# Retention scores with the key halves of odd chunks exchanged in PSUM, and three steps placed elsewhere

## What is computed

```python
def _attn_ref(q, k, v):                      # q, k, v: (2, 8, 768, 64)
    gamma = 1.0 - 2.0 ** (-5.0 - arange(H))
    for t in range(S):
        state = gamma * state + k[t] (outer) v[t]
        y[t] = q[t] @ state / sqrt(D)

def _moe_ref(x, g_ln, w_ch1, w_ch2):         # x: (2, 768, 512), y with its heads side by side
    xn = (x - mean(x)) / sqrt(var(x) + 1e-6) * g_ln
    return x + relu(xn @ w_ch1) @ w_ch2
```

## Time and profile before

| what | value |
|---|---|
| median of 3 executions | 446.19 us (446.08 to 446.53) |
| profiled execution, its own time | 447.54 us |
| span of the profiled execution | 445.8 us |
| TensorE busy | 439.6 us, 99% of the span |
| VectorE busy | 316.7 us, 71% |
| ScalarE busy | 227.5 us, 51% |
| GpSimd busy | 291.4 us, 65% |
| granted TensorE clock | 1.00 of full speed |

### The profile page before, as it was taken

The page is one execution under the profiler, slowest core; times in us unless marked ns, Lnnn a source line. Parts: engine busy times, 40 slices in busy tenths (PEclk is TensorE's granted clock), DMA queues, the critical chain, the costliest instruction groups (busy, mean ns, idle before and its releaser), DMA issues.

```text
span 445.8 us, 8757 instructions
## 1 busy us (share of the span) xinstructions
PE 439.6 (99%) x3150; PEld 400.0 (90%) x3150; DVE 316.7 (71%) x670; ACT 227.5 (51%) x531; POOL 291.4 (65%) x390
## 2 busy tenths in 40 slices
PE   7999999999999999999999999999999999999997
PEld 7899988989898899898989898988999999999886
DVE  2655889767876857776786677648557888887963
ACT  3458965532451465444245234215436777777853
POOL 2856845989788599997876696632803355566650
PEclk9999999999999999999999999999999999999999
DMA  8999304221211311331132260020163533333214
GB/s 206 253 264 258 119 0 143 56 84 50 96 51 49 91 33 63 94 96 48 49 94 62 81 164 4 0 49 1 25 152 78 141 94 97 93 97 89 89 49 165
DMA packets 68474, 41.52 MB, mean 93 GB/s; under 512 B 35792, under 2 KB 62672, under 8 KB 68432
## 3 DMA queue, kind: packets, MB, share of 16 engines
q1 hardware_dynamic: 66288, 40.37, 33.3%
q10 hardware_dynamic: 2144, 0.60, 0.6%
HBM read 28.37 MB, written 3.15 MB: 71 GB/s over the span
## 4 chain that ended last, share of the span: by engine, by line
PE 95%; DVE 1%; DMA 1%; ACT 1%; issue 1%; ACTq 0%; DVEq 0%
PE ps L988 30%; PE ps L969 25%; PE ps L1104 8%; PE ps L1123 4%; PE ps L1157 4%; PE ps L1138 4%; PE ps L1074 4%; PE ps L1193 3%; PE ps L823 3%; PE ps L812 3%; PE ps L835 3%; PE ps L928 2%; PE ps L881 1%; PE ps L848 1%; DMA decay_sb<-decay 1%; PE ps L1086 1%
## 5 line engine op out<-in xcount | busy, mean ns | idle before, releaser
L1388 ACT ACTIVATE h_t_hi<-ps 128x384 fp32r<-128x384 f32 x64 | 31.3, 490 | 126.2 <-DVE ps L1742 68.2
L988 PE MATMUL ps<-w_hi,h_t_lo 128*128 128x512 f32 x192 | 76.1, 397 | 0.0
L988 PE MATMUL ps<-w_lo,h_t_hi 128*128 128x512 f32 x192 | 75.8, 395 | 0.0
L988 PE MATMUL ps<-w_hi,h_t_hi 128*128 128x512 f32 x192 | 74.7, 389 | 0.0
L681 POOL TENSOR_TENSOR w_lo<-raw_w,w_hi 128x512 fp32r<-128x512 f32 x32 | 43.1, 1369 | 40.0 <-ACT w_hi L1335 30.4
L772 POOL TENSOR_SCALAR a<-a,inv_den,weight 128x768 f32<-128x768 f32 (+5 forms) x48 | 34.0, 718 | 52.5 <-DVE inv_den L1984 28.0
L1723 DVE SCALAR_TENSOR_TENSOR h_t_lo<-ps,h_t_hi 128x384 fp32r<-128x384 f32 x64 | 35.6, 556 | 32.6 <-ACT h_t_hi L1388 32.6
L666 POOL TENSOR_TENSOR w_lo<-w_sum,w_hi 128x256 fp32r<-128x256 f32 x60 | 45.1, 762 | 2.4
L988 PEld LDWEIGHTS ps<-w_hi,h_t_lo 128*128 128x128 f32 x192 | 36.0, 187 | 7.7
L1476 ACT ACTIVATE a<-a,neg_max 128x768 f32<-128x768 f32 (+5 forms) x48 | 32.2, 674 | 16.9 <-DVE neg_max L1965 16.9
L969 PE MATMUL ps<-xq_T_lo,w_hi 128*128 128x384 f32 x120 | 40.6, 338 | 0.0
(11 more groups left out here) (206 smaller groups left out, 1193.5 us busy)
## 6 DMA issues: line engine op xcount, KB each, us to landing
raw_w<-in_moe_w_ch SPq DMA_DIRECT2D x64, 256.0 KB, 2.9
k_twice_hi<-pj_hi SPq DMA_DIRECT2D x32, 96.0 KB, 2.2
k_twice_lo<-pj_lo SPq DMA_DIRECT2D x32, 96.0 KB, 2.2
out_y<-out_sb SPq DMA_DIRECT2D x11, 256.0 KB, 2.0
raw_k<-in_k SPq DMA_DIRECT2D x7, 384.0 KB, 5.8
raw_q<-in_q SPq DMA_DIRECT2D x7, 384.0 KB, 5.9
raw_v<-in_v SPq DMA_DIRECT2D x7, 384.0 KB, 5.2
q_both<-pj_hi SPq DMA_DIRECT2D x16, 96.0 KB, 2.1
```

The lines of the kernel that those rows point to most:

```text
L988: mm = pe.matmul(acc_bank(tau), h_tile(a_, m, which)[:, u * P:(u + 1) * P], w2[b_][:, m % 2, part, :], start=(m % NG == 0 and which in ("1 ...
L1388: act.activation(h_tile("hi", m, part), part_bank(m, part), ACT.Relu).then_inc(s_hhi, 1)
```

## The change

1. In `scores_of` the result of key half 0 of an odd chunk goes to PSUM partitions 64 to 127 and that of half 1 to 0 to 63; even chunks stay as they were. Which chunk of a group is odd depends on the group: the middle one in group 0, the outer two in group 1.
2. `apply_causal` becomes three instructions for each group in place of one: one for the even chunks, and for the odd chunks one for each half, which reads the PSUM half on the other side and writes the half of `prob` where it belongs. The block of the odd chunks that is always zero is no longer written there.
3. GpSimd prepares a second form of the triangle in `causal`, and clears the zero block of `prob` with four memsets, before it starts to scale. VectorE waits for this (`s_const` at 10 in place of 4).
4. `scale_last("q")` stands ahead of all four first `weight_lo` in GpSimd's list; it stood between the second and the third.
5. The four `centre` of batch 0 stood ahead of `states(6)`. Now two stand behind `states(6)` and two behind `states(7)`.

```diff
-            pool.memset(causal[:, :], 1.0).then_inc(s_const, 1)
+            pool.memset(causal[:, :, :], 1.0).then_inc(s_const, 1)
             pool.wait_ge(s_const, 3)
...
+            pool.affine_select(out=causal[:, 1, 0:D], in_=causal[:, 1, 0:D], compare_op=ALU.is_ge, fill=0.0, base=D,
+                               pattern=[[1, D]], channel_multiplier=-1).then_inc(s_const, 1)
+            pool.affine_select(out=causal[0:D, 1, D:P], in_=causal[0:D, 1, D:P], compare_op=ALU.is_ge, fill=0.0, base=0,
+                               pattern=[[1, D]], channel_multiplier=-1).then_inc(s_const, 1)
+            pool.wait_ge(s_const, 6)
+            for it in range(2):
+                for g in range(2):
+                    pool.memset(prob[head_rows(1), it, g, :, odd_chunks(g), 0:D], 0.0).then_inc(s_const, 1)
+            pool.wait_ge(s_const, 10)
...
             scale_last("k")
-            for name in FIRST_WEIGHTS[:2]:
-                weight_lo(0, name)
             scale_last("q")
-            for name in FIRST_WEIGHTS[2:]:
+            for name in FIRST_WEIGHTS:
                 weight_lo(0, name)
...
                         seen = slice(half * D, P)
+                        place = head_rows(half if c % 2 == 0 else 1 - half)
                         for j in range(2):
-                            mm = pe.matmul(s_bank(g)[head_rows(half), j, c % G, seen], k_t(c)[head_rows(j), head_rows(half)],
+                            mm = pe.matmul(s_bank(g)[place, j, c % G, seen], k_t(c)[head_rows(j), head_rows(half)],
...
-                dve.tensor_tensor(prob[:, it % 2, g], s_bank(g),
-                                  causal[:, :].unsqueeze(1).unsqueeze(1).broadcast_to((P, 2, G, P)),
-                                  ALU.mult).then_inc(s_prob, 1)
+                chunks = even_chunks(g)
+                count = len(range(G)[chunks])
+                dve.tensor_tensor(prob[:, it % 2, g, :, chunks, :], s_bank(g)[:, :, chunks, :],
+                                  causal[:, 0, :].unsqueeze(1).unsqueeze(1).broadcast_to((P, 2, count, P)), ALU.mult)
+                chunks = odd_chunks(g)
+                count = G - count
+                for half in range(2):
+                    seen = slice(half * D, P)
+                    mask = causal[head_rows(1 - half), 1, seen].unsqueeze(1).unsqueeze(1)
+                    masked_rows = dve.tensor_tensor(prob[head_rows(half), it % 2, g, :, chunks, seen],
+                                                    s_bank(g)[head_rows(1 - half), :, chunks, seen],
+                                                    mask.broadcast_to((D, 2, count, P - half * D)), ALU.mult)
+                masked_rows.then_inc(s_prob, 1)
...
-            dve.wait_ge(s_const, 4)
+            dve.wait_ge(s_const, 10)
...
-                if it == HP + 2:
-                    for kk in range(KT):
-                        centre(0, 0, kk)
                 states(it)
+                if it in (HP + 2, HP + 3):
+                    for kk in range(2):
+                        centre(0, 0, 2 * (it - HP - 2) + kk)
```

More of the change, by code:

```diff
@@ L119, in retention_moe_program @@
         mean_of = sb(ctx, "mean_of", [P, P], F32R)
-        causal = sb(ctx, "causal", [P, P])
+        causal = sb(ctx, "causal", [P, 2, P])
         masked = sb(ctx, "masked", [P, NC, P], BF16)
@@ L314, in y_rows, with even_chunks, odd_chunks @@
             return head_rows(1 - j if g == 1 else j)
+        def even_chunks(g):
+            return slice(g, G, 2)
+        def odd_chunks(g):
+            return slice(1 - g, G, 2)
         def part_of(g):
@@ L631, in _ @@
             diagonal(ident)
-            pool.memset(causal[:, :], 1.0).then_inc(s_const, 1)
+            pool.memset(causal[:, :, :], 1.0).then_inc(s_const, 1)
             pool.wait_ge(s_const, 3)
-            pool.affine_select(out=causal[:, :], in_=causal[:, :], compare_op=ALU.is_ge, fill=0.0, base=0,
+            pool.affine_select(out=causal[:, 0, :], in_=causal[:, 0, :], compare_op=ALU.is_ge, fill=0.0, base=0,
                                pattern=[[1, P]], channel_multiplier=-1).then_inc(s_const, 1)
+            pool.affine_select(out=causal[:, 1, 0:D], in_=causal[:, 1, 0:D], compare_op=ALU.is_ge, fill=0.0, base=D,
[7 more added lines that the diff above has]
+            pool.wait_ge(s_const, 10)
             pool.tensor_scalar(mean_of[:, :], ident[:, :], 0.0, 1.0 / DM, ALU.mult, ALU.add).then_inc(s_const, 1)
             pool.memset(masked[:, :, :], 0.0).then_inc(s_const, 1)
-            pool.wait_ge(s_const, 6)
+            pool.wait_ge(s_const, 12)
             pool.affine_select(out=masked[:, NC - 1, :], in_=masked[:, NC - 1, :], compare_op=ALU.is_ge, fill=MASKED, base=0,
@@ L856, in first_mean @@
             def first_mean(b):
-                pe.wait_ge(s_const, 5)
+                pe.wait_ge(s_const, 11)
                 if b == 1:
```

## The result

The change makes the kernel slower. After it the median is 452.23 us (451.62 to 452.83, four runs), beside 446.36 us (446.08 to 447.37, four runs) for the kernel before. The ratio is 1.0127, with a 95% interval of 1.0103 to 1.0151, so 5.9 us more. The profiled execution took 452.74 us with a span of 451.0 us and a mean granted clock of 0.996.

A forecast was written before the change was run, and what follows sets the result against it. TensorE, with 95% of the chain, was taken to bound the kernel. first_mean(1) shifts 4.9 us, 2.2 by pair 7 and 2.7 waiting for tiles; from the median 446.19 that gives 451.1 us, range 448.2 to 453.2.

The forecast's parts named there:

- The mean's shift: TensorE's first_mean(1) moves from 56.74 to 61.6 us, +4.9: 2.2 came in with pair 7, 2.7 from waiting for tiles.
- a rival at 0.15: TensorE falls to its lower clock around the late mean, costing 2 us more: 453.1 us; chance 0.15.
- 1, the exchange: TensorE's scores stages, with records spread evenly over the column halves, get at most 0.32 us shorter for each pair.
- The rival that the exchange gives nothing in any pair: TensorE's scores get no shorter in any pair: 0.7 us more, 451.8 us; chance 0.05.
- 2, the masks: VectorE's masks of a pair, three instructions a group with gaps between, take 3.05 us in place of 1.82.
- The rival of 2.4 us: VectorE's new masks overlap as now and take 2.4 us a pair: +2.3 us, 448.5 us; chance 0.10.
- 3, pair by pair: TensorE's shifts: pair 0 +1.0 us, pair 1 +0.8, pairs 2 to 5 -0.3, pair 5 +0.7; 2.2 at pair 7.
- 4, the centre tiles: ScalarE's quad_hi B21 waits for tiles 2 and 3, holding outputs the mean needs: +2.7 us; TensorE idle about 1.8.
- 5, at nothing: GpSimd's new constants and the earlier last q scaling cost nothing; the four weight_lo keep their sum.
- The sum: Span 445.8 + 4.9 = 450.7 us for the profiled execution; from the median of 446.19, 451.1 us.

The follow-up runs named there:

- exchange_alone: Kernel before with only TensorE's exchange of the odd chunks' halves, masks left as one instruction, so outputs are wrong: 445.35 us, ratio 0.9983.
- masks_alone: Kernel after with three mask instructions a group but no exchange: 450.33, 450.49 and 450.58 us at clock 1.000, 453.69 at 0.992; ratio 1.0118.
- first_two_whole: Kernel after with pairs 0 and 1 neither exchanged nor masked in three instructions: 448.67, 448.70 and 449.46 us at clock 1.000, 450.10 at 0.995.
- q_scaling_alone: Kernel before with only GpSimd's last q scaling moved ahead of the first two weight_lo: 446.27 us, ratio 0.9999.
- head_copies_first: Kernel after with ScalarE's head output copies of pairs 6 and 7 ahead of quad_hi B21, the low-priority weights' copies ahead of both: 448.94 us, ratio 1.0060.
- centre_back: Kernel after with all four centre tiles back ahead of states(6), as in the kernel before: 448.99 us, ratio 1.0066.
- old_pool_order: Kernel after with the last q scaling back behind the first two weight_lo: median 451.11 us; one run of four, 453.51 us, at clock 0.992.
- gap_filled: Kernel after with twelve unread identity transposes in TensorE's idle time ahead of mean(1): 450.53 us, clock 0.999 or 1.000 in all four runs.
- turned_rows: Kernel before with the exchange made in the loads of k and v from pair 1 on, masks kept at two a pair: 452.95 us, ratio 1.0151.

## Why the prediction was right

The forecast was 451.1 us (448.2 to 453.2), slower at 0.88. The time is 452.23 us. The mean's shift, the main term, was 4.9 us and measured 4.76. That it is so near is in part luck: up to pair 7's masks I had 0.4 us too much, and from there to the mean 0.2 too little. The rest of the difference is a rival at 0.15 that came true. The mean stands at 60.66 us in the trace, not at 61 to 62, since the scores of pair 0 began 0.84 us sooner than in the trace of before. By its steps:

- **1, the exchange.** Stage of pair 6 shorter by 0.29 us, for "at most 0.32". In pairs 3 to 5 I took 0.1 a pair, and the rows give 0.2. The mechanism is right, and its size is shown alone by exchange_alone: 1.0 us. The rival that the exchange gives nothing in any pair is wrong. Whether its gain outlives the longer masks is open: masks_alone reached the mean 0.37 us sooner without it, but its sums in pair 5 were 0.58 us shorter.
- **2, the masks.** 3.05 us forecast, 3.02 measured, with gaps of 0.02 or more between them. The rival of 2.4 us fell.
- **3, pair by pair.** The sum at pair 1 was 1.8 and measured 1.2 in the trace (13.44 for 12.24), where the exchange of pair 2 is in it; first_two_whole has the masks and the exchange of the two pairs together at 1.69. The 2.20 us of pair 0's scores belonged to that execution: q_scaling_alone has the same 48 records in 1.72, and the kernel after in 1.62. Pairs 2 to 4 gave back 0.58 and not 0.3. For pair 5 I had 0.7 and it was 1.09 (7.41 for 6.32). The mechanism named, ScalarE's rounded sum coming late, is there, but TensorE meets it in `first_mean(0)` first, where it waited 1.27 us. The step had no term for the GpSimd operations that these sums wait for: the sum took 0.83 us, for 0.55, and `sums_lo` 0.99, for 0.55 too. At pair 7's masks it is +1.74 (42.29 for 40.55) and I had 2.1. The errors of this step cancel in part.
- **4, the centre tiles.** Forecast 2.7 us in this stretch, measured 3.2 from pair 6's chunk outputs (8.96 for 5.74) and 3.0 from pair 7's masks (9.91 for 6.89). The idle time of ScalarE (3.64 us) and of TensorE ahead of the mean (1.70, for about 1.8) are as forecast, and head_copies_first and centre_back show the cause. That the first products start late was forecast without a size, and TensorE waits 0.91 us for them. Not forecast is its wait of 0.27 us ahead of its last state outputs, for states that come behind the masks. Neither lies on the way to the mean.
- **5, at nothing.** Shown for the q scaling by q_scaling_alone. The new constants were not tested alone.
- **The sum.** It left out the clock. I took 453.1 us as the time with a fall, at 2 us a fall, and gave it 0.15; it came in all four runs, at 1.36 us in the profiled one. Without it this kernel would be at about 450.9 us: 452.23 less 1.36. The step that failed is that chance. I had "no row decides", and the one that bore on it was my own of step 4: a TensorE that works 1 us out of 3.7. Even so four falls in four runs are partly chance: old_pool_order has the same gap, and one in four.

## What to carry to other kernels

Count the instructions a faster stage puts on its neighbour, and where that neighbour's list sets the next meeting point; the stage's own gain is set against that (0.2 us a pair here, for 1.2 us more of masks). An operation that waits for late data holds up all that stands behind it in its engine's list, so put what the critical path needs ahead of it: that alone was worth 3.3 us, the clock's fall that it avoided among them. When a change opens a gap on TensorE of a microsecond or two with little work around it, price the lower clock too. And where a short VectorE operation lies on the way, look what GpSimd has running when it starts: the same sum took 0.55 to 1.22 us here.

## What the runs showed of the hardware

- The granted clock fell in some executions of a kernel and not in others. It did so where TensorE was busy 2.05 of 4 us (after) or 1.44 of 4 us (old_pool_order), but masks_alone had 1.53 of 4 in its profiled run and kept its clock there, and in three runs of four. In gap_filled, with 3.01 of 4, it fell in none of four. It cost 1.36 us with a mean clock of 0.996 and 2.84 us at 0.992. What decides between the runs stays open: the traces don't show it.

The Trainium skill (TensorE: Matmul & The Clock Gate, What's actually happening) says that the array runs at 1.2 GHz unless recent activity has released it. The rows agree that in some executions it returns there after a stretch with little work (0.50 from 60 to 62 us in old_pool_order).

- A 384-column sum of VectorE took 0.55 or 0.56 us when no GpSimd operation was running at its start, and otherwise ended no sooner than 0.40 us after that operation, up to 1.22 us in all (98 sums in 14 traces, in either order of GpSimd's list). It rests on these times; no kernel was run with GpSimd's work taken away.
- On a full queue, 96 KB of v over 64 partitions landed in 4.7 us and 192 KB over 128 partitions in 4.3 us; for k both took 4.0 us (medians of turned_rows).
